# First expert's tokens gathered by TensorE with 0/1 matrices beside the sort through DRAM

## The chip, the core and the metric

The kernel runs on one core of a Trainium2 chip. A core has TensorE (PE, matrix products, with its weight loads shown apart as PEld), VectorE (DVE), ScalarE (ACT), GpSimd (POOL) and SyncE (SP, which here only issues transfers). The metric is the device time of one execution in microseconds, the median of several runs.

## What is computed

Causal attention with a decay (2 batches, 8 heads, 576 positions, 64 columns each), then a mixture of eight experts with one expert for each of the 1152 tokens, then a dense two-layer product. The part that matters here is the mixture:

```python
logits = x @ w_gate                                   # 1152 x 512 by 512 x 8
expert_idx = np.argmax(logits, axis=1)
gate_w = softmax(logits)[arange(N), expert_idx]
for i in range(N):                                    # at most 288 tokens an expert
    e = expert_idx[i]
    if counts[e] < capacity:
        disp[e, counts[e]] = x[i]; pos[i] = counts[e]; counts[e] += 1; keep[i] = True
y = np.einsum('ecf,efd->ecd', np.maximum(np.einsum('ecd,edf->ecf', disp, w1), 0.0), w2)
out[i] = gate_w[i] * y[expert_idx[i], pos[i]]         # 0 where not kept
```

Each expert has w1 of 512x1024 and w2 of 1024x512.

## The kernel before

Every engine has a program of its own, written out by hand, and runs it in order; semaphores join them. Each float32 product is made of three: operands are split into a high part in fp32r and the rest (`hi`, `lo`), and TensorE computes hi*hi, lo*hi and hi*lo (L704, L705 and L706, `expert_product`).

**Attention** leaves in `xl` (in SBUF) the rows of all heads and their share of the logits. The 1152 tokens lie in 10 tiles (`TILES`) of 128 or 64 tokens.

**Routing** (from L1081) is a chain of short VectorE instructions. `onehot` (L1091) marks each token's expert; TensorE counts with `tri_b` and `ones_b` how many tokens of each expert stand before each token (L678 to L683); from `bank(0)` and `bank(1)` VectorE works out `starts` (where each expert begins in the sorted order), `dest` (each token's sorted place) and `scale` (its gate, 0 if dropped). `r_dest` and `r_side` tell the others.

**Sorting through DRAM.** The 10 tiles of scaled rows `xr` are made by VectorE (even tiles, L1131) and ScalarE (odd, L862). GpSimd scatters each with an indirect DMA to its place in `x_scratch` (L438). When all ten have landed, SP reads them back as 9 tiles `x_sorted` (L371). TensorE transposes each with four matmuls (`sorted_t`, L693), and ScalarE or VectorE copies the result into `x_t`. Three tiles (`FIRST_T`) hold the first expert's 288 columns: they come first, are split into `xe` (hi by ScalarE at L888, lo by VectorE at L1157), and expert 0 starts. The other six are transposed one behind each output tile `m` of expert 0's first layer. While TensorE has nothing to do it runs `spin`, products of ones that nobody reads: 98 of them ahead of the first transposed tile (L494).

**Experts.** `expert(e)` runs 8 output tiles of the first layer with 12 matmuls each, then 96 matmuls of the second layer, in the order kk 0 to 3 over all four m, then m by m over kk 4 to 7. ScalarE and VectorE take each hidden tile out of PSUM (L905, L1149), split the next weights (`cut_hi`, L271; `cut_lo`, L278; chunk 3 is w2's second half of expert 0, 4 and 5 are w1 of expert 1), and make the next expert's `xe`. `cut_x_hi` and `cut_x_lo` read the expert's start from `starts` into a register first. After expert 0 GpSimd zeroes `y_t` (L444), for which the first `y_high` waits (`pads`).

## Time and profile before

| | us |
|---|---|
| median of 3 runs | 589.86 (588.75 to 591.75) |
| the profiled execution, device time | 588.54 |
| its span, first to last instruction | 586.7 |
| attention, and the routing's counts done | to 140.8 |
| expert 0's first matmul | at 169.96 |
| expert 1's first matmul | at 198.17 |

Times in the trace are counted from the span's start. "Idle before" of a group is the time its engine stood still just ahead of it, with the engine and instruction that ended the wait. Matmuls overlap, so that the time between two starts, and not the duration of one, is what a matmul costs.

### The profile page before, as it was taken

Reading aid. Unit: us, or ns where it says so; the run is one execution under the profiler, and the core shown is the slowest. Engines: PE = TensorE matmul, PEld = TensorE weight load, DVE = VectorE, ACT = ScalarE, POOL = GpSimd, SP = SyncE. Lnnn points to the kernel's source line nnn. Section 1 sums busy time; section 2 is a strip of 40 time slices with the busy share of each in tenths; the row PEclk is TensorE's granted clock in tenths of the full one; section 3 lists DMA queues with packets and bytes.
Section 4 is the critical chain, followed back from the end, with each engine's and each line's share of the span. In section 5 each row is a group of like instructions: output and inputs, shape, how many; then the busy total and the mean of one; then the engine's idle time right before and its main releaser. Section 6 shows DMA issues by size and latency. Waiting matters only on the chain.

```text
span 586.7 us, 9523 instructions
## 1 busy us (share of the span) xinstructions
PE 568.8 (97%) x3694; PEld 504.0 (86%) x3694; DVE 327.5 (56%) x648; ACT 286.3 (49%) x571; POOL 60.0 (10%) x65
## 2 busy tenths in 40 slices
PE   7999999999989999999999999989999999999993
PEld 3688888886469999999999999979999898999992
DVE  4777777876124584665747556776333534353432
ACT  4677777762125364463735446655232323333330
POOL 7311111100702400000000000000000200010001
PEclk8999999999999999999999999999999999999998
DMA  8996563120460444626355462642000100000001
GB/s 167 228 276 179 165 153 85 69 73 2 164 235 0 144 155 181 215 97 216 114 174 185 175 216 73 216 144 73 0 1 1 54 1 1 2 33 22 1 0 54
DMA packets 51212, 63.63 MB, mean 108 GB/s; under 512 B 30496, under 2 KB 30528, under 8 KB 51168
## 3 DMA queue, kind: packets, MB, share of 16 engines
q1 hardware_dynamic: 48272, 57.34, 31.8%
q0 software_dynamic: 1520, 4.77, 2.2%
q10 hardware_dynamic: 1376, 0.92, 0.6%
q8 instruction: 29, 0.48, 0.4%
q14 instruction: 15, 0.12, 0.1%
HBM read 58.25 MB, written 4.77 MB: 107 GB/s over the span
## 4 chain that ended last, share of the span: by engine, by line
PE 90%; DVE 3%; POOL 2%; DMA 2%; issue 1%; ACT 1%; SPq 0%; DVEq 0%; ACTq 0%
PE ps L704 12%; PE ps L705 12%; PE ps L706 11%; PE ps L778 6%; PE ps L779 6%; PE ps L780 5%; PE ps L761 5%; PE ps L763 5%; PE ps L762 5%; PE ps L533 4%; PE ps L515 4%; PE ps L558 3%; PE ps L552 3%; PE ps L502 2%; POOL x_scratch L438 2%
## 5 line engine op out<-in xcount | busy, mean ns | idle before, releaser
L278 DVE TENSOR_TENSOR slot<-stage,slot 128x1024 fp32r<-128x1024 f32 x80 | 95.4, 1221 | 21.1 <-ACT slot L271 20.9
L930 ACT ACTIVATE act_t<-ps,half 128x384 f32<-128x384 f32 x48 | 27.9, 582 | 115.1 <-PE ps L763 115.1
L271 ACT ACTIVATE slot<-stage 128x1024 fp32r<-128x1024 f32 x80 | 81.4, 1052 | 4.6 <-DMA stage<-in_moe_w_in_dram 2.6
L1205 DVE SCALAR_TENSOR_TENSOR act_t<-act_t 128x384 f32<-128x384 f32 x48 | 26.8, 559 | 98.6 <-ACT act_t L930 98.6
L704 PE MATMUL ps<-xe,slot 128*128 128x288 f32 x256 | 75.8, 296 | 0.3 <-DVE xe L1157 0.3
L705 PE MATMUL ps<-xe,slot 128*128 128x288 f32 x256 | 75.6, 295 | 0.0
L705 PE MATMUL ps<-hid,slot 128*128 128x288 f32 x256 | 75.6, 295 | 0.0
L706 PE MATMUL ps<-xe,slot 128*128 128x288 f32 x256 | 75.3, 294 | 0.0
L706 PE MATMUL ps<-hid,slot 128*128 128x288 f32 x256 | 75.3, 294 | 0.0
L704 PE MATMUL ps<-hid,slot 128*128 128x288 f32 x256 | 75.2, 294 | 0.0
L905 ACT ACTIVATE hid<-ps 128x288 fp32r<-128x288 f32 x64 | 26.4, 412 | 99.7 <-PE ps L706 98.8
L761 PE MATMUL ps<-y_t,slot 128*128 128x384 f32 x192 | 64.8, 338 | 0.0
L763 PE MATMUL ps<-y_t,slot 128*128 128x384 f32 x192 | 64.6, 336 | 0.0
L762 PE MATMUL ps<-y_t,slot 128*128 128x384 f32 x192 | 64.4, 335 | 0.0
L1149 DVE SCALAR_TENSOR_TENSOR hid<-ps,hid 128x288 fp32r<-128x288 f32 x64 | 29.1, 454 | 60.9 <-ACT hid L905 60.9
L778 PE MATMUL ps<-slot,g_t 128*128 128x512 f32 x144 | 56.7, 394 | 1.9 <-DVE g_t L1213 1.9
L779 PE MATMUL ps<-slot,g_t 128*128 128x512 f32 x144 | 56.6, 393 | 0.0
L780 PE MATMUL ps<-slot,g_t 128*128 128x512 f32 x144 | 56.0, 389 | 0.0
L704 PEld LDWEIGHTS ps<-xe,slot 128*128 128x128 f32 x256 | 48.3, 189 | 0.8 <-DVE xe L1157 0.8
L706 PEld LDWEIGHTS ps<-xe,slot 128*128 128x128 f32 x256 | 48.4, 189 | 0.0
L706 PEld LDWEIGHTS ps<-hid,slot 128*128 128x128 f32 x256 | 48.4, 189 | 0.0
L704 PEld LDWEIGHTS ps<-hid,slot 128*128 128x128 f32 x256 | 48.3, 189 | 0.0
(163 smaller groups left out, 1054.4 us busy)
## 6 DMA issues: line engine op xcount, KB each, us to landing
stage<-in_moe_w_dram SPq DMA_DIRECT2D x32, 1024.0 KB, 5.2
cb<-c_scratch SPq DMA_DIRECT2D x7, 576.0 KB, 4.0
x_sorted<-x_scratch SPq DMA_DIRECT2D x9, 258.0 KB, 5.0
q_nat<-in_q_dram SPq DMA_DIRECT2D x16, 128.0 KB, 3.6
v_nat<-in_v_dram SPq DMA_DIRECT2D x16, 128.0 KB, 4.0
stage<-in_moe_w_in_dram SPq DMA_DIRECT2D x2, 1024.0 KB, 5.3
stage<-in_moe_w_out_dram SPq DMA_DIRECT2D x2, 1024.0 KB, 5.9
stage<-in_moe_w_in_dram SPq DMA_DIRECT2D x4, 512.0 KB, 5.1
```

The source lines that it names most:

```text
L271: nc.scalar.activation(s[:, 0, at], stages[n_buf][:, at], ACT.Copy).then_inc(w_hi, 1)
L278: nc.vector.tensor_tensor(s[:, 1, at], stages[stage_of(g)[0]][:, at], s[:, 0, at].bitcast(F32), ALU.subtract).then_inc(w_lo, 1)
L704: mm(bank(b, CAP), hi, x[:, 0], start=first, stop=False)
L705: mm(bank(b, CAP), lo, x[:, 0], start=False, stop=False)
L706: return mm(bank(b, CAP), hi, x[:, 1], start=False, stop=last)
L761: mm(bank(j % 2, TC), hi, y_t[:, 0, kk, TC * c:TC * c + TC], start=(kk == 0), stop=False)
L762: mm(bank(j % 2, TC), hi, y_t[:, 1, kk, TC * c:TC * c + TC], start=False, stop=False)
L763: last = mm(bank(j % 2, TC), lo, y_t[:, 0, kk, TC * c:TC * c + TC], start=False, stop=(kk == KD - 1))
L778: mm(b, gh, hi, start=(j == 0), stop=False)
L779: mm(b, gh, lo, start=False, stop=False)
L780: last = mm(b, gl, hi, start=False, stop=(j == NJ - 1))
L1149: V.scalar_tensor_tensor(out=hid[:, m, 1], in0=bank(m % 4, CAP), scalar=0.0, in1=hid[:, m, 0].bitcast(F32), op0=ALU.max, op1=ALU.subtract) ...
```

## The change

Expert 0's tokens no longer come from DRAM. Four pieces replace that:

- `sel`: ten 128x288 matrices of 0 and 1, made by GpSimd with a comparison of `slot_f` (0 to 287 in a row) with `place0`, the token's place within expert 0 (`before` of expert 0, plus 4096 for tokens of other experts). `slot_f` is made by two GpSimd instructions at the program's start.
- `sx`: the rows of each tile times the gate, split into hi (ScalarE) and lo (VectorE), six buffers deep.
- TensorE multiplies them (`select`): 4 matmuls of 128x288 for each tile and part, 80 in all, into banks 4 to 7, which then hold expert 0's rows selected and transposed. The lo part of a tile is taken `SLAG` (4) tiles behind its hi part.
- ScalarE and VectorE split the four banks into `xe`.

The scaled rows `xr` are still made, between the pieces of `sx`; GpSimd's ten scatters stand behind its ten comparisons. All nine sorted tiles are now transposed within expert 0's second layer, at the places of `SORT_AT`, into banks 0 to 3. The cuts of chunk 3 stand behind hidden tiles 2 and 4, those of chunks 4 and 5 between the copies of sorted tiles, and expert 1's `xe` last. The zeroing of `y_t` is in two halves.

Core of the diff:

```diff
+SXR, SLAG = 6, 4
...
+        SORT_AT = {(1, 3): [0, 1], (2, 3): [2, 3], (3, 3): [4, 5], (7, 0): [6, 7], (7, 1): [8]}
...
             # GpSimd
+            step(g.iota(slot_i[:], pattern=[[1, CAP]], base=0, channel_multiplier=0))
+            step(g.tensor_copy(slot_f[:], slot_i[:]))
...
+            pool.wait_ge(places0, 2)
+            for i in range(TILES):
+                g.tensor_scalar(sel[:, i], slot_f[:], small[:, 10, i:i + 1], None, ALU.is_equal).then_inc(sel_sb, 1)
             pool.wait_ge(r_dest, 1)
...
+            pool.wait_ge(x0_ps, KD)
+            g.memset(y_t[:, 1].bitcast(F32), 0.0).then_inc(pads, 1)
             pool.wait_ge(xt_ps, ST)
             pool.wait_ge(idx_sb, 1)
-            g.memset(y_t[:].bitcast(F32), 0.0).then_inc(pads, 1)
+            g.memset(y_t[:, 0].bitcast(F32), 0.0).then_inc(pads, 1)
...
             # TensorE
+            spin(4, 3)
+            def select(i, part):
+                pe.wait_ge(sx_hi if part == 0 else sx_lo, i + 1)
+                if part == 0:
+                    pe.wait_ge(sel_sb, i + 1)
+                for kk in range(KD):
+                    last = mm(bank(4 + kk, CAP), sx[:, i % SXR, part, P * kk:P * kk + P], sel[:, i],
+                              start=(i == 0 and part == 0), stop=(i == TILES - 1 and part == 1))
...
+            for i in range(TILES + SLAG):
+                if i < TILES:
+                    select(i, 0)
+                if i >= SLAG:
+                    select(i - SLAG, 1)
...
-            spin(98, 3)
-            for t in range(FIRST_T):
-                sorted_t(t)
-                spin(4, 3)
-            spin(10, 3)
...
+                        if e == 0 and m == 0:
+                            pe.wait_ge(x0_lo, kk + 1)
...
-                    if e == 0 and FIRST_T + m < ST:
-                        sorted_t(FIRST_T + m)
...
+                    if e == 0:
+                        for t in SORT_AT.get((kk, m), []):
+                            sorted_t(t)
...
             # ScalarE
+            act.wait_ge(gates, 1)
+            for i in range(TILES):
+                select_hi(i)
+                if i in (4, 6, 7, 8, 9):
+                    scaled_rows({4: 1, 6: 3, 7: 5, 8: 7, 9: 9}[i])
...
+            for kk in range(KD):
+                act.wait_ge(x0_ps, kk + 1)
+                A.activation(xe[:, kk, 0], bank(4 + kk, CAP), ACT.Copy).then_inc(x0_hi, 1)
...
             # VectorE
+            V.tensor_scalar(off0, onehot[:, :, 0], -4096.0, 4096.0, ALU.mult, ALU.add).then_inc(places0, 1)
             then(V.reduce_sum(total, by_tile(expo), AX_X))
             then(V.tensor_scalar(total, total, 1.0e-9, None, ALU.add))
+            V.reciprocal(gate, total).then_inc(gates, 1)
...
+            V.tensor_tensor(place0, before.rearrange("p (t e) -> p t e", t=TILES)[:, :, 0], off0, ALU.add).then_inc(places0, 1)
...
-            V.reciprocal(gate, total).then_inc(r_side, 1)
...
+            for i in range(TILES):
+                select_lo(i)
+                if i % 2 == 0:
+                    scaled_rows(i)
+            for kk in range(KD):
+                dve.wait_ge(x0_hi, kk + 1)
+                V.tensor_tensor(xe[:, kk, 1], bank(4 + kk, CAP), xe[:, kk, 0].bitcast(F32), ALU.subtract).then_inc(x0_lo, 1)
...
                 if e == 0:      # ScalarE; VectorE has the like with tiles 1, 3, 5, 7
+                    cut_hi(4, 0)
+                    cut_hi(4, 1)
+                    sorted_copy(0)
+                    sorted_copy(2)
+                    cut_hi(5, 0)
+                    sorted_copy(4)
+                    cut_hi(5, 1)
+                    sorted_copy(6)
+                    sorted_copy(8)
+                    cut_x_hi(1)
+                    continue
```

TensorE, from the counts on, before (`xs_in0` is the landing of the first sorted tile):

```order
L683 MATMUL ps<-onehot,ones_b 128x8 x10
L494 MATMUL ps<-ones_b 128x512 x98
L693 MATMUL ps<-ident,x_sorted 128x128 [waits xl_sb,xs_in0]
L693 MATMUL ps<-ident,x_sorted 128x128 x3
L494 MATMUL ps<-ones_b 128x512 x4
```

and now:

```order
L699 MATMUL ps<-onehot,ones_b 128x8 x10
L510 MATMUL ps<-ones_b 128x512 x4
L709 MATMUL ps<-sel,sx 128x288 [waits sel_sb,sx_hi,xl_sb]
L709 MATMUL ps<-sel,sx 128x288 x3
L709 MATMUL ps<-sel,sx 128x288 [waits sel_sb,sx_hi]
```

In the place of 98 spins and the wait for DRAM stand four spins and the selecting matmuls, which wait for the comparisons and for `sx`.

VectorE behind the routing chain, before:

```order
L1127 CAST starts<-small 128x8
L1131 TENSOR_SCALAR xr<-xl,small 128x512 [waits r_side]
L1131 TENSOR_SCALAR xr<-xl,small 128x512 x4
L278 TENSOR_TENSOR slot<-stage,slot 128x1024 [waits w_hi,w_st0]
L278 TENSOR_TENSOR slot<-stage,slot 128x1024 [waits w_hi]
```

and now:

```order
L1190 CAST starts<-small 128x8
L1198 SCALAR_TENSOR_TENSOR sx<-xl,small,sx 128x512 [waits sx_hi]
L1206 TENSOR_SCALAR xr<-xl,small 128x512 [waits r_side]
L1198 SCALAR_TENSOR_TENSOR sx<-xl,small,sx 128x512 [waits sx_hi] x2
L1206 TENSOR_SCALAR xr<-xl,small 128x512
```

and so on to the tenth lo part. The five scaled rows now stand between ten lo parts, and the cuts of chunk 3 have moved into expert 0.

ScalarE after expert 0's last hidden tile, now (before, the cuts of chunks 4 and 5 stood behind `xe`, and the copies of sorted tiles in the first layer):

```order
L951 ACTIVATE hid<-ps 128x288 [waits h_ps] x3
L278 ACTIVATE slot<-stage 128x1024 [waits h_ps,w_st1]
L278 ACTIVATE slot<-stage 128x1024
L923 ACTIVATE x_t<-ps 128x4x128 [waits xt_ps] x2
L278 ACTIVATE slot<-stage 128x1024 [waits h_ps,w_st2]
L923 ACTIVATE x_t<-ps 128x4x128 [waits xt_ps]
```

against before:

```order
L905 ACTIVATE hid<-ps 128x288 [waits h_ps] x2
L887 TENSOR_LOAD starts [waits pads,xt_a,xt_v]
L887 ISA x2
L888 ISA
L888 ACTIVATE xe<-x_t 128x4x288
L271 ACTIVATE slot<-stage 128x1024 [waits h_ps,w_st1]
```

Expert 1's `xe` has moved behind the last sorted tile's copy.

## Rows read from the trace of the kernel before

**Rows 1.** The page: busy us, share of the span and instructions of each engine.

```profile
PE 568.8 (97%) x3694; PEld 504.0 (86%) x3694; DVE 327.5 (56%) x648; ACT 286.3 (49%) x571; POOL 60.0 (10%) x65
```

**Rows 2.** A stretch's busy us by engine, clock, DMA; then TensorE's waits (us, times, longest).

```profile
198.00:300.00 102.00, 102.00 (x774) 102.00 (x773) 61.84 (x72) 51.84 (x72) 0.00 (x0) 1.00 0.49 167
...
PE ps L778 <- DVE g_t L1213: 1.9, 2, 1.6
```

**Rows 3.** The chain that ended last, 140 to 170: start us, us, what.

```profile
140.81 0.18 DVE small L1105
...
145.32 1.25 POOL x_scratch L438
...
157.98 2.60 DMA x_scratch<-xr,dest
160.59 2.74 DMA x_sorted<-x_scratch
...
169.96 0.40 PE ps L704
```

**Rows 4.** TensorE in order of time: first matmuls of expert 1 and expert 2.

```profile
198.17 0.29 PE L704 MATMUL ps<-xe,slot 128*128 128x288 f32 x1
...
223.56 0.29 PE L704 MATMUL ps<-xe,slot 128*128 128x288 f32 x1
```

**Rows 5.** ScalarE and VectorE: two timeline rows, then groups (busy, mean ns | idle before).

```profile
143.85 3.18 ACT L862 ACTIVATE xr<-xl,small 128x512 f32<-128x512 f32 x5 [4.43 <-DVE starts L1127]
...
143.96 2.07 DVE L1131 TENSOR_SCALAR xr<-xl,small 128x512 f32<-128x512 f32 x5
...
L988 DVE TENSOR_TENSOR pt<-ps,pt 128x512 fp32r<-128x512 f32 x16 | 10.3, 684 | 0.0
...
L905 ACT ACTIVATE hid<-ps 128x288 fp32r<-128x288 f32 x64 | 26.4, 412 | 99.7 <-PE ps L706 98.8
...
L1149 DVE SCALAR_TENSOR_TENSOR hid<-ps,hid 128x288 fp32r<-128x288 f32 x64 | 29.1, 454 | 60.9 <-ACT hid L905 60.9
```

**Rows 6.** GpSimd's elementwise groups; the last with min/median/max ns.

```profile
L429 POOL CAST vs<-v_nat 128x640 fp32r<-128x640 f32 x8 | 5.7, 716 | 79.1 <-PE ps L552 58.2 <-DMA v_nat<-in_v_dram 20.8
...
L414 POOL CAST erank<-erank_i 128x80 f32<-128x80 int32 x1 | 1.3, 1325 | 0.1
...
L395 POOL CAST ident_b<-ident 128x128 bf16<-128x128 f32 x1 | 0.3, 289 | 0.1
...
L431 POOL TENSOR_TENSOR vs<-v_nat,vs x8: 1545/1549/2460, 14.6 to 110.9; 128x640 fp32r<-128x640 f32 x8
```

**Rows 7.** VectorE and GpSimd at work at once, two places in the timeline.

```profile
14.27 1.47 DVE L1017 TENSOR_TENSOR_SCAN xl<-sc,xl 16x576 f32<-16x576 f32 x1
...
14.62 2.46 POOL L431 TENSOR_TENSOR vs<-v_nat,vs 128x640 fp32r<-128x640 f32 x1
...
148.08 2.36 DVE L278 TENSOR_TENSOR slot<-stage,slot 128x1024 fp32r<-128x1024 f32 x2 [2.05 <-ACT slot L271]
...
148.17 1.96 POOL L438 DMA_INDIRECT x_scratch<-xr,dest  x1 [0.31 <-issue]
```

**Rows 8.** TensorE's first transposes and the wait ahead; that stretch as in rows 2.

```profile
8.71 1.30 PE L502 MATMUL ps<-ident,q_nat 128*128 128x128 f32 x5 [2.61 <-DMA q_nat<-in_q_dram]
...
8.00:12.00 4.00, 3.29 (x14) 2.60 (x15) 2.76 (x3) 2.28 (x4) 2.96 (x8) 0.57 1.19 160
```

**Rows 9.** Expert 1's `xe` in the timeline, and the copies of sorted tiles (min/median/max ns).

```profile
186.61 1.17 ACT L888 ACTIVATE xe<-x_t 128x1152 fp32r x1 [0.52 <-issue]
...
188.83 1.36 DVE L1157 TENSOR_TENSOR xe<-x_t,xe 128x1152 fp32r<-128x1152 f32 x1 [2.13 <-issue]
...
L869 ACT ACTIVATE x_t<-ps x5: 597/597/598, 164.1 to 182.5; 128x512 f32<-128x512 f32 x5
```

**Rows 10.** Reading back: SP's issues in the timeline, and from issue to landing.

```profile
160.59 4.48 SPq L371 DMA_DIRECT2D x_sorted<-x_scratch  x9
...
DMA to landing us min/median/max: 2.7/5.0/5.7
```

More of the change, by code:

```diff
@@ L692, in sorted_t @@
                 for kk in range(KD):
[L693 removed]
+                    last = nc.tensor.transpose(bank(t % 4, P, P * kk), x_sorted[:, t, P * kk:P * kk + P], ident[:])
                 last.then_inc(xt_ps, 1)
[L696 to L700 removed]
             def expert_product(b, hi, lo, x, first, last):
@@ L1075, in _ @@
             best, total, gate = row(3, TILES), row(4, TILES), row(5, TILES)
+            off0, place0 = row(9, TILES), row(10, TILES)
             pick9 = small[:, 6:8, :].rearrange("p a c -> p (a c)")[:, 0:TILES * (E + 1)].rearrange("p (t e) -> p t e", t=TILES)
```

124 lines of the change are left out of this document (76 added, 48 removed).

## The prediction

> **What bounds the kernel now.** The page first: TensorE is busy for 97% of the span, VectorE for 56% and ScalarE for 49% [rows 1]. That share has to be read by stage, since TensorE also spins there. From 198 us on it is really bound by its matmuls: it is busy for all of the 102 us after 198, and of all its waits behind that the view of waits lists 1.9 us [rows 2]. What brings expert 1 forward therefore brings the end forward by as much, as long as weights and splits keep up. The chain of waits then shows the one stage in which TensorE does nothing of use: the counts are out at 140.81, GpSimd scatters from 145.32 to about 158, the last scatter lands at 160.59, and expert 0 begins at 169.96 [rows 3]; between the first two the routing's chain ends at 143.96, where the scaled rows start [rows 5]. That is 29.15 us from the counts to expert 0, filled by spins.
>
> **Routing, now.** VectorE gets `off0` and `place0` ahead of its chain, some 0.15 us each, and loses the reciprocal from its middle. I count nothing: the chain still ends at about 143.96. The gate is ready by 140.9, so ScalarE starts `sx` hi at 141.0. GpSimd starts comparing at about 141.1.
>
> **Feeding the selection.** ScalarE: five scaled tiles took 3.18 us, and so (3.18 - 0.71) / 4 = 0.62 us each in a row [rows 5]. It has 10 hi parts and 5 scaled tiles; the tenth hi part is its 14th instruction, starts at 141.0 + 13 x 0.62 = 149.1 and ends at 149.8. VectorE: a scaled tile costs (2.07 - 0.48) / 4 = 0.40 us in a row. A 128x512 operation with two tensors takes 0.684 us [rows 5]; taking off the overlap of 0.08 that the scaled tiles show, 0.60 in a row. The tenth lo part starts at 143.96 + 9 x 0.60 + 5 x 0.40 = 151.4 and ends at 152.1. TensorE: 96 matmuls for a layer and 192 for an expert take 223.56 - 198.17 = 25.39 us [rows 4], 0.132 each, of the same 128x288 form. The 80 selecting ones are 10.6 us, 0.53 for a tile and part. With the interleaving, the last five groups follow the tenth hi part: 149.9 + 6 x 0.53 = 153.1. TensorE and VectorE end nearly together, at about 153.
>
> **GpSimd's comparison** is not in the trace: bounds. Below, its one-input rows: 0.289 us for 128 columns and 0.716 for 640 [rows 6], which is 0.83 ns a column and 0.42 us for 288. Above, by its two-input row, 1.549 for 640 [rows 6], 0.85 us with the same fixed part. The operation has one tensor, so I take 0.42: the tenth is done by 145.3. TensorE needs it at 149.9; it may take up to 0.88 us before it is late. The two new instructions at the start of the program lie ahead of work that has several microseconds of cover, and cost nothing.
>
> **GpSimd and VectorE in each other's way.** This is the term that I would have missed from durations alone. At 14.62 GpSimd's operation took 2.46 us for a usual 1.55, while VectorE was in a scan with two inputs from SBUF until 15.74; and the scatter at 148.17 took 1.96 us beside VectorE's subtraction at 148.08, which also reads two tensors from SBUF [rows 6, 7]. The lo parts of `sx` and some eight small steps of the routing chain read two tensors from SBUF, while GpSimd compares. Bounds: nothing, if only GpSimd gives way; and 2.6 us if each gives way to the other: eight steps wait for half a comparison (8 x 0.2 = 1.6) and the remaining two or three comparisons hold a lo part each (1.0). The first row is nearer to a full block of GpSimd (0.91 of the 1.12 us that the scan still ran); for VectorE it shows no clear loss. I take 1.5 us. The Trainium skill ("SBUF — State Buffer", section "SBUF: two separate sides") says that VectorE and GpSimd share a pair of ports under an exclusive lock, held for the whole instruction, and that the loser blocks fully. The trace agrees for GpSimd, with the 2.46 us; for VectorE no row decides. By the page the 2.6 us would hold, and the time would be 1.1 us above my forecast.
>
> **Into expert 0.** Behind the last selecting matmul of the first bank stand a ScalarE copy (0.41) and a VectorE subtraction (0.45) of 128x288 [rows 5], where there were copies of 1152 columns; the next three banks follow while TensorE computes. Without contention expert 0 runs as if begun at 153.1 + 0.9 = 154.0, against 169.96: 16.0 us. Contention takes it to 155.5.
>
> **Inside expert 0.** Before, expert 0 took 198.17 - 169.96 = 28.21 us, with six transposed tiles: (28.21 - 25.39) / 6 = 0.47 each. Now all nine are in it: 25.39 + 9 x 0.47 = 29.6. It costs 1.4 us, and matmuls end at 155.5 + 29.6 = 185.1.
>
> **The new wait.** Expert 1's `xe` now waits for the ninth sorted tile, which is transposed ahead of the last 24 matmuls. Behind it: the completion and ScalarE's copy, 0.15 + 0.60; the start's load, 0.52; hi, 1.17; from its end at 187.78 to VectorE's start at 188.83, with VectorE's own load, 1.05; lo, 1.36 [rows 9]. Together 4.9 us, against 24 x 0.132 = 3.2 of cover. TensorE stands still for 1.7 us (I hold 1.2 to 2.3 possible). Expert 1 begins at 186.8.
>
> **What stays hidden.** The scatters stand behind the comparisons and last 157.98 - 145.32 = 12.7 us to the last issue [rows 3]. With VectorE's lo parts in their way I let them begin at 147 and lose 2 more: the last lands at about 164.5, the first sorted tile at 167.2, the last at 164.5 + 4 + 5 = 173.5 [rows 10]. TensorE wants them at 155.5 + 12.7 + 3.2 = 171.4 and at about 181.5. 4 us of cover. Chunk 3's cuts are wanted at about 174; chunks 4 and 5 lie in the second layer, where ScalarE and VectorE have room.
>
> **The sum.** Selection instead of sorting -16.0; contention +1.5; three more transposed tiles +1.4; the wait before expert 1 +1.7: -11.4 us. From there on TensorE is the bound as before. Against the profiled execution, 588.54 (span 586.7), this gives 577.1; that execution lies 1.3 us under the median, and against the median of 589.86 it gives 578.5.
>
> **Rivals.**
> *The comparisons are slow.* If one takes 1.0 to 1.5 us (the two-input price of 0.85 plus blocks by VectorE), the tenth is done at 151 to 156.1, and TensorE still has 6 groups behind it: expert 0 is 0 to 5 us later, up to 583. For it: the bound is only twice what I take. Against: one tensor.
> *Sorted tiles late.* If the scatters are held up by over 4 us more than I count, the wait moves into the second layer: each us over it costs one; 580 to 584. For it: rows 7. Against: VectorE is through with lo parts at 153.
> *The clock falls.* The spins also kept TensorE at 2.4 GHz. Once it fell, to a mean of 0.57, after TensorE had stood still for 2.6 us at the start [rows 8]. If it ran at 1.2 GHz through the selection, 80 matmuls would take 21 us, and expert 0 would begin near 163.7: 586 to 587. Against: it gets 0.53 us of matmuls in each 0.62.
> *Slower than before.* One GpSimd row is out of line: a conversion of 80 columns took 1.325 us, 16.6 ns a column [rows 6]. A comparison at that price takes 4.8 us, the tenth ends at 189, and expert 0 begins at 193: 616. It decides from 2.2 us each, where the gain is gone. Against: that one broadcasts its input over ten short rows, and is the only one.
> *Nothing moves*, because something else holds expert 1 back to 198: no row speaks for it, as before its `xe` was ready 8 us ahead.
>
> **How the numbers follow.** Forecast 0.67, slow comparisons 0.13, late tiles 0.08, clock 0.04, slower 0.05, nothing 0.03. About 0.5% (3 us) is what a measurement can tell from no change here. The low end is no contention and a short new wait: 578.5 - 1.5 - 1.0 - 0.5 for the runs' spread, 575.5. The high end takes in slow comparisons and late tiles up to 583.5; what lies above holds less than 2 in 10. Faster 0.92, same 0.03, slower 0.05.
>
> **What would show it.** In the profile after: selecting matmuls from 141.7 to 153 or 155, at a clock of 1.0; the comparisons at 0.4 us each when alone, and VectorE's small steps stretched beside them; expert 0's first matmul at 154 to 156; a TensorE wait of 1 to 2 us for VectorE's `xe` before expert 1; none for `x_sorted`. A comparison of over 0.9 us, a wait at `x_sorted`, or a clock under 1 in the selection would make me wrong.

## The result and the profile after

| | before | after |
|---|---|---|
| median, us | 590.74 (588.75 to 593.09, 5 runs) | 584.35 (583.73 to 587.01, 5 runs) |
| the profiled execution, device time | 588.54 | 584.01 |
| its span | 586.7 | 581.9 |
| expert 0's first matmul | 169.96 | 157.64 |
| expert 0's second layer | 185.48 | 172.66 |
| expert 1's first matmul | 198.17 | 191.53 |
| expert 2's first matmul | 223.56 | 218.58 |

The ratio is 0.9915, 95% interval 0.9889 to 0.9941: about 0.9% faster. The time lies 5.9 us over the forecast of 578.5 and just above the range (575.5 to 583.5). A gain of 11.4 us was forecast, and 5.0 came through, read at expert 2. The difference to the prediction is therefore 6.4 us, and it has to be found ahead of 218.58. Behind it nothing is new: from expert 2's start to the end are 363.3 us, before 363.1.

The page of the kernel after, busy us by engine (to be held against [rows 1]):

```profile
PE 559.2 (96%) x3658; PEld 505.5 (87%) x3658; DVE 336.9 (58%) x663; ACT 292.6 (50%) x584; POOL 72.2 (12%) x78
```

GpSimd has 12.2 us more. The chain of waits of the kernel after, from the counts to expert 0 (start us, us, what; answers to [rows 3]):

```profile
140.73 0.16 DVE small L1168
...
140.98 4.78 POOL sel L445 x5
145.76 0.69 issue
146.45 5.60 POOL sel L445 x4
...
152.19 4.29 PE ps L709 x29
...
156.59 0.42 ACT xe L919
...
157.03 0.47 DVE xe L1215
...
157.64 0.37 PE ps L736
```

No transfer stands in this chain any more, and GpSimd's comparisons fill 10.4 us of its 16.9. The 0.69 us called "issue" is no pause: the fifth comparison is recorded from 144.93 to 146.47, and its increment of `sel_sb` at 146.48. The timeline of the same stretch (start us, busy us, instruction, idle time before and what ended it):

```profile
140.85 3.17 ACT L900 ACTIVATE sx<-xl,small 128x512 fp32r<-128x512 f32 x5 [1.44 <-DVE small L1159]
140.98 12.32 POOL L445 TENSOR_SCALAR sel<-slot_f,small 128x288 fp32r<-128x288 f32 x10 [28.54 <-DVE small L1168]
...
144.55 0.74 DVE L1198 SCALAR_TENSOR_TENSOR sx<-xl,small,sx 128x512 fp32r<-128x512 f32 x1
...
145.60 1.57 DVE L1198 SCALAR_TENSOR_TENSOR sx<-xl,small,sx 128x512 fp32r<-128x512 f32 x2
...
153.47 1.23 POOL L452 DMA_INDIRECT x_scratch<-xr,dest  x1 [0.17 <-issue]
```

The tenth comparison ends at 153.3 instead of the 145.3 that I had forecast, and behind it stand the six groups of matmuls of the interleaving and the two copies: expert 0 begins 4.34 us later. VectorE's first lo part starts at 144.55 instead of 143.96.

Then the stages of expert 0 and 1, of the kernel after (stretch, busy us by engine, clock, DMA share, GB/s; the rows are expert 0's first layer, its second layer with the wait, and expert 1):

```profile
157.64:172.66 15.02, 13.66 (x97) 13.02 (x98) 5.66 (x11) 4.60 (x10) 12.48 (x9) 1.00 0.62 206
172.66:191.53 18.87, 16.88 (x135) 16.64 (x133) 9.95 (x13) 8.37 (x11) 4.91 (x1) 1.00 0.67 230
191.53:218.58 27.05, 27.05 (x193) 27.05 (x193) 15.55 (x18) 12.95 (x18) 0.00 (x0) 0.94 0.41 133
```

An expert's layer is 96 matmuls, 12.7 us [rows 4]. The first layer took 15.02 and lost 2.3 (the same layer of expert 0 takes 12.76 in an execution shown below). The second layer's matmuls, with nine transposed tiles, end at 189.37, 16.71 us behind its start, of which 12.69 are its own and 4.02 the tiles': 0.45 each, as predicted. Expert 1 took 27.05 us where [rows 4] have 25.39; its clock shows why, 0.94 on average. Four places, then: the start of expert 0 (2.1 us late), its first layer (2.1 over the forecast, since its matmuls took 31.73 us in all instead of 29.6), the wait before expert 1 (0.5 over), and expert 1's own clock (1.7).

Expert 1's `xe` in the timeline of the kernel after:

```profile
186.36 0.60 ACT L923 ACTIVATE x_t<-ps 128x512 f32<-128x512 f32 x1 [1.86 <-PE ps L731]
...
187.89 1.18 ACT L935 ACTIVATE xe<-x_t 128x1152 fp32r x1 [0.93 <-ACT x_t L923]
...
190.12 1.36 DVE L1234 TENSOR_TENSOR xe<-x_t,xe 128x1152 fp32r<-128x1152 f32 x1 [5.00 <-issue]
...
191.53 0.40 PE L736 MATMUL ps<-xe,slot 128*128 128x288 f32 x1 [1.99 <-DVE xe L1234]
```

Between two matmuls' starts TensorE had a gap of 2.28 us here, and 1.1 us behind it the granted clock was 0.50 from 192.6 to 196.0.

### The profile page after: what moved, and what is told of

It is laid out like the page before. It is cut to its first block, busy times and chain, and to the rows that moved or that the text cites. A ratio compares the mean times of both kernels' runs of the same rounds, so it can differ in the third digit from the quotient of the medians.

```text
span 581.9 us, 9504 instructions
## 1 busy us (share of the span) xinstructions
PE 559.2 (96%) x3658; PEld 505.5 (87%) x3658; DVE 336.9 (58%) x663; ACT 292.6 (50%) x584; POOL 72.2 (12%) x78
## 4 chain that ended last, share of the span: by engine, by line
PE 89%; DVE 2%; POOL 2%; issue 2%; ACT 1%; DMA 1%; another core or an unknown queue 1%; SPq 0%; DVEq 0%; ACTq 0%
PE ps L736 11%; PE ps L737 11%; PE ps L738 11%; PE ps L813 6%; PE ps L814 6%; PE ps L815 6%; PE ps L796 5%; PE ps L798 5%; PE ps L797 5%; PE ps L549 4%; PE ps L531 4%; PE ps L574 3%; PE ps L568 3%; POOL sel L445 2%; PE ps L518 2%
## 5 line engine op out<-in xcount | busy, mean ns | idle before, releaser
L464 POOL DMA_INDIRECT out_dram<-o_sb,tok_sorted x9 | 9.0, 995 | 377.6 <-DVE o_sb L1283 376.7
L736 PEld LDWEIGHTS ps<-xe,slot 128*128 128x128 f32 x256 | 49.0, 191 | 4.4 <-DVE xe L1234 2.2
L737 PEld LDWEIGHTS ps<-xe,slot 128*128 128x128 f32 x256 | 48.6, 190 | 0.8 <-issue 0.8
L738 PEld LDWEIGHTS ps<-xe,slot 128*128 128x128 f32 x256 | 49.0, 192 | 0.0
## 6 DMA issues: line engine op xcount, KB each, us to landing
cb<-c_scratch SPq DMA_DIRECT2D x7, 576.0 KB, 3.7
```

Source lines behind the costliest of these rows:

```text
L736: mm(bank(b, CAP), hi, x[:, 0], start=first, stop=False)
L737: mm(bank(b, CAP), lo, x[:, 0], start=False, stop=False)
L738: return mm(bank(b, CAP), hi, x[:, 1], start=False, stop=last)
```

## The experiments

The result is the first of five series. Fifteen more runs make the other four, each on one chip beside the kernel before. Three of the runs are the kernel after again, since what a single execution shows turned out to matter. "First layer" below is always expert 0's.

### The half clock behind the wait

**Spins in the wait.** Nine products of ones, ahead of the wait for expert 1's `xe`:

```diff
             for e in range(E):
+                if e == 1:
+                    pe.wait_ge(xt_v, 3)
+                    spin(9, 1)
                 if e >= 1:
                     pe.wait_ge(xe_lo, e)
```

> Nine spins (about 1.9 us of products that nobody reads) stand ahead of TensorE's wait for expert 1's xe. In the changed kernel that wait lasted 2.2 us, behind it the granted clock was half for 3.4 us, and expert 1 took 27.05 us against 25.39 before. Theory clock: the standstill made the clock fall; with spins it stays at full, expert 1 takes 25.4, and the time is 1.7 us under the changed kernel's. Rival: the slow stretch belongs to expert 1's place in time or to its load, not to the standstill; the clock falls all the same and the time doesn't move (or rises by the spins that run over, at most 0.3).

Measured: 580.31 us (580.16 to 583.23, 4 runs), ratio 0.9842 (0.979 to 0.9894), span 578.1. The stretch behind the wait, in the kernel after (stretch, busy us by engine, clock, DMA share, GB/s):

```profile
192.60:196.00 3.40, 3.40 (x17) 3.40 (x16) 1.00 (x2) 1.35 (x2) 0.00 (x0) 0.50 0.00 0
```

and the same in the kernel with spins, where expert 1 is by then 2.2 us further:

```profile
192.60:196.00 3.40, 3.40 (x28) 3.40 (x27) 2.27 (x4) 1.79 (x4) 0.00 (x0) 1.00 0.00 0
```

17 matmuls at 1.2 GHz against 28 at 2.4. Expert 1 took 25.5 us (189.30 to 214.82). The spins shorten nothing, as expert 1 still waits for its `xe`; only the half clock is gone. The rest of the difference to 581.9 is the first layer, which took 12.80 here. By itself this execution does not show that the spins did it, since the kernel without them also runs without the half clock at times, as the next lines tell.

Whether the clock falls behind this wait differs between executions. Eleven of those profiled have a gap of 2.26 to 2.30 us there. In seven (the first of the kernel after, and `plain_pool`, `scatter_late`, `sel_split`, `price`, `plain_fourth`, `late_fourth` below) a half-clock stretch of 3.4 us begins within 1.1 us of the gap's end; in four (`sel_alone` and the three later ones of the kernel after) none does. In none of the six executions without the gap (`before`, `spin_wait`, `sort_early`, `best`, `slag2`, `best2`) is there one before expert 1. It is this count, seven of eleven against none of six, that ties the half clock to the gap. The length of the gap does not tell the seven from the four. So the wait costs some 2.2 us, and in more than half of the executions 1.7 on top.

### What sets expert 0's start

**Comparisons alone.** VectorE's first lo part waits for all ten comparisons:

```diff
             def select_lo(i):
+                if i == 0:
+                    dve.wait_ge(sel_sb, TILES)
                 dve.wait_ge(sx_hi, i + 1)
```

> VectorE's first lo part waits for all ten comparisons, so that no operation with two tensors from SBUF runs beside the last six. In the changed kernel the first four comparisons took 1.00 us each and the last six 1.42. Theory price plus contention: all ten take 1.0 us, the tenth ends at 151.0 instead of 153.3, and lo parts take 0.74 us each with none at 0.9 or 1.0. Rival price alone: the later ones still take 1.25 or more, from ScalarE or TensorE at work beside them. The time itself will be higher, as lo parts start at 151 and end at 159: expert 0 at about 160.5.

Measured: 588.45 us (one execution), expert 0 at 166.04 instead of the expected 160.5. Two half-clock stretches put it back: one from 135.7 to 142.5, ahead of the change, and one from 152.7 to 159.6, which began within TensorE's 5.11 us before the first lo part. GpSimd's prices are not touched by that. The comparisons of this kernel (count, ns least/median/most, first and last start):

```profile
L445 POOL TENSOR_SCALAR sel<-slot_f,small x10: 990/991/1015, 144.0 to 152.9; 128x288 fp32r<-128x288 f32 x10
```

and those of the kernel after:

```profile
L445 POOL TENSOR_SCALAR sel<-slot_f,small x10: 997/1262/1565, 141.0 to 152.0; 128x288 fp32r<-128x288 f32 x10
```

By itself a comparison takes 0.99 us, more than my upper bound of 0.85. In the kernel after the first four take 1.00 to 1.02 beside VectorE's short steps, and the six beside lo parts 1.24 to 1.56. The lo parts give way too: in `sel_alone` all ten took 0.74 to 0.75 us, in the kernel after up to 0.99:

```profile
L1198 DVE SCALAR_TENSOR_TENSOR sx<-xl,small,sx x10: 739/742/991, 144.5 to 153.7; 128x512 fp32r<-128x512 f32 x10
```

Together the ten take from 140.98 to 153.3, 12.3 us; in `sel_alone` they take 9.82, one behind the other. Contention costs some 2.4 us on the path. The rival is out: the fifth and sixth comparison of `sel_alone` ran beside TensorE's and ScalarE's work (up to 149.7 and 149.3), and took 0.99 too. The Trainium skill ("SBUF — State Buffer", section "SBUF: two separate sides") says that the loser of the shared ports waits for the whole instruction. The direction agrees, on both engines here; the losses are 0.25 to 0.57 us for a comparison and up to 0.25 for a lo part, and don't tell whether a block is ever a whole instruction long.

**What the price hangs on.** Twelve instructions on GpSimd where TensorE does not wait for it, twice six forms:

```diff
             pool.wait_ge(x0_ps, KD)
+            g.memset(y_t[:, 1].bitcast(F32), 0.0).then_inc(probe, 1)
...
+                        last = g.tensor_scalar(dst, src, one, None, ALU.is_equal)
...
+                        last = g.tensor_scalar(dst, src, 1.0, None, ALU.is_equal)
...
+                        last = g.tensor_scalar(dst[:, 0:144], src[:, 0:144], one, None, ALU.is_equal)
...
+                        last = g.tensor_scalar(dst[:, 0:72], src[:, 0:72], one, None, ALU.is_equal)
...
+                        last = g.tensor_copy(dst, src)
...
+                        last = g.tensor_scalar(dst, src, 1.0, None, ALU.mult)
```

> The changed kernel with twelve more GpSimd instructions, twice six forms one behind the other, at a place where TensorE does not wait for GpSimd (behind the zeroing of half of y_t, in expert 0's first layer): the comparison with its threshold from SBUF on 288, 144 and 72 columns, the comparison with a constant, a copy and a multiplication by a constant on 288 columns. Theory A, the price is per column: 0.99 us for 288, 0.50 for 144, 0.25 to 0.30 for 72, and the copy takes 0.42 as worked out from the conversion's rows. Theory B, a fixed price of the form with a threshold from SBUF: 144 and 72 columns take nearly as long as 288, and the comparison with a constant is shorter. Some of the twelve may be longer where VectorE works on two tensors beside them; the shorter of each pair counts.

Measured, in one execution, by line (L465 the form of `sel`, L467 with a constant, L469 and L471 with 144 and 72 columns, L473 the copy, L475 the multiplication):

```profile
L465 POOL TENSOR_SCALAR y_t<-y_t x2: 1013/1018/1022, 175.5 to 181.8; 128x288 fp32r<-128x288 f32 x2
...
L467 POOL TENSOR_SCALAR y_t<-y_t x2: 1914/1942/1969, 176.6 to 182.9; 128x288 fp32r<-128x288 f32 x2
...
L469 POOL TENSOR_SCALAR y_t<-y_t x2: 647/814/980, 178.6 to 184.9; 128x144 fp32r<-128x144 f32 x2
...
L471 POOL TENSOR_SCALAR y_t<-y_t x2: 463/782/1102, 179.7 to 185.6; 128x72 fp32r<-128x72 f32 x2
...
L473 POOL CAST y_t<-y_t x2: 425/426/428, 180.2 to 186.8; 128x288 fp32r<-128x288 f32 x2
...
L475 POOL TENSOR_SCALAR y_t<-y_t x2: 935/941/947, 180.7 to 187.3; 128x288 fp32r<-128x288 f32 x2
```

The copy of 288 columns takes 0.43 us, which is the 0.42 that I had worked out from conversions, to the hundredth. The interpolation was right, the kind of instruction was not: a multiplication by a constant on the same columns already takes 0.94, and the comparison 1.01. With 72, 144 and 288 columns it is 0.46, 0.65 and 1.01, about 0.28 us and 2.5 ns a column. Theory A holds in its main point (a price by the column) with a fixed part that it did not have. The Trainium skill ("GPSIMD Engine Reference", section "Engine selection") calls GpSimd's elementwise operations with one input roughly line-rate; the copy here is in keeping with it, the multiplication and the comparison on the same columns, at over twice the time, are not. The long ones of a pair, and both of L467, stand beside one of VectorE's subtractions of two tensors (1.22 us each) and are 0.3 to 0.95 longer; for the comparison with a constant this experiment therefore gives no price of its own.

**Split between two engines.** VectorE makes the five odd ones ahead of the rest of its chain:

```diff
-            for i in range(TILES):
+            for i in range(0, TILES, 2):
                 g.tensor_scalar(sel[:, i], ...)
...
             V.tensor_tensor(place0, ...)
+            dve.wait_ge(places0, 2)
+            for i in range(1, TILES, 2):
+                V.tensor_scalar(sel[:, i], slot_f[:], small[:, 10, i:i + 1], None, ALU.is_equal).then_inc(sel_v, 1)
```

> The five odd comparisons are made by VectorE, ahead of the rest of its routing chain, the five even ones by GpSimd. Theory (GpSimd's ten comparisons at 1.0 to 1.6 us set the start of expert 0): GpSimd is through at about 146.5, VectorE's five take 0.25 to 0.35 us each (1.2 to 1.8 us together) and put its chain back by that, and its lo parts become the bound: expert 0 begins at 155.0 to 156.0 instead of 157.6, and the time falls by 1.6 to 2.6. Rival (what VectorE gives away in its chain and its lo parts costs as much): expert 0 begins at 157 or later and nothing is gained. The wait before expert 1 stays at about 2.2 us.

Measured: 582.13 us (580.76 to 584.23, 4 runs), ratio 0.9881 (0.9848 to 0.9915); the kernel after beside it had 580.25. The rival was right. GpSimd was through at 146.4, but VectorE's five took 2.44 us, its first lo part started at 146.37, and TensorE stood still for 2.06 us until it was there. From 149.0 to 152.4 the clock was half, and expert 0 began at 158.18. The half clock explains a part of that: 13 matmuls of the selection went at 0.24 us each instead of 0.13, 1.4 us. Without it, by my estimate from these starts, expert 0 would begin near 156.8, still behind the 155.0 to 156.0 of the theory, as the last lo part ended only at 155.07. TensorE in the timeline of this kernel:

```profile
142.51 2.88 PE L710 MATMUL ps<-sel,sx 128*128 128x288 f32 x20 [0.76 <-ACT sx L901]
147.16 0.80 PE L710 MATMUL ps<-sel,sx 128*128 128x288 f32 x4 [1.78 <-DVE sx L1202]
```

and the stretch of the selection (columns as before; the clock is 0.90 on average):

```profile
141.00:158.00 17.00, 13.68 (x84) 12.40 (x82) 14.18 (x40) 10.64 (x18) 13.88 (x9) 0.90 0.10 39
```

So VectorE is the next bound close behind the comparisons; in the kernel after its last lo part ends at 154.4, 1.1 us behind the last comparison.

### The late hidden tiles of the first layer

**The kernel after once more:**

> The changed kernel as it is, profiled a second time. In its first profiled execution expert 0's first layer took 15.02 us and TensorE stood still for 2.3 us in it, because ScalarE was told of three finished hidden tiles some 5 us late; in four variants that layer took 12.8. Theory A, an event of that one execution: the first layer takes 12.7 to 12.8 us here, and the span is about 579.6 (581.9 - 2.3) with the half clock behind the wait for expert 1's xe, 577.9 without. Theory B, it belongs to this kernel: 15.0 again and a span near 582. In both, the ten comparisons take 1.0 us alone and 1.2 to 1.6 beside VectorE's lo parts, and expert 0 begins at 157.6.

Measured: 580.25 us (580.05 to 585.38, 4 runs), ratio 0.9873 (0.9828 to 0.9918), spans 578.1, 578.2, 578.2 and 583.3. ScalarE's second to fourth hidden tile in this execution:

```profile
161.11 0.41 ACT L951 ACTIVATE hid<-ps 128x288 fp32r<-128x288 f32 x1 [1.18 <-PE ps L738]
162.70 0.41 ACT L951 ACTIVATE hid<-ps 128x288 fp32r<-128x288 f32 x1 [1.18 <-PE ps L738]
...
164.28 0.41 ACT L951 ACTIVATE hid<-ps 128x288 fp32r<-128x288 f32 x1 [0.23 <-PE ps L738]
```

and the second to fifth in the first execution:

```profile
162.83 0.41 ACT L951 ACTIVATE hid<-ps 128x288 fp32r<-128x288 f32 x1 [2.92 <-issue]
167.85 0.41 ACT L951 ACTIVATE hid<-ps 128x288 fp32r<-128x288 f32 x1 [4.62 <-remote]
...
169.11 0.70 ACT L951 ACTIVATE hid<-ps 128x288 fp32r<-128x288 f32 x2
```

Here tiles come every 1.585 us and the first layer takes 12.76. In the first execution the third tile must have been finished near 162.7, too, since TensorE ran without a gap until 165.9; but its increment of `h_ps` is recorded at 167.83, with those of the next two behind it at 167.96 and 168.08. There is a second trace of it: ten scatters with sixteen increments each make 160 of `x_out`. This execution has all 160, the first one 48, and the last of the 48 is at 167.54, just ahead of the late increments (171.00 and 171.03 in `after_third`; but in `slag2` below the late ones come at 169.4 and the last of the scatters' at 170.3). The clock did not fall either, where I had expected it half behind the wait.

What TensorE itself lost in the first execution is mostly not a wait for a late hidden tile. Its longest gap there:

```profile
165.91 0.29 PE L738 MATMUL ps<-xe,slot 128*128 128x288 f32 x1
167.10 0.29 PE L736 MATMUL ps<-xe,slot 128*128 128x288 f32 x1 [0.90 <-issue]
```

and the one of `slag2`:

```profile
168.64 0.29 PE L738 MATMUL ps<-xe,slot 128*128 128x288 f32 x1 [0.80 <-issue]
```

The program waits for hidden tiles (`h_lo`) only ahead of a tile's twelve matmuls. These gaps lie between the third and fourth, and between the eleventh and twelfth, matmul of the sixth tile, where it waits for nothing. In the first execution two such gaps (1.19 and 0.46 between starts) cost 1.4 us; the gaps ahead of the seventh and eighth tile (0.33 and 0.56), where TensorE does wait for late hidden tiles, cost 0.6. In `price` and `slag2` one gap in the sixth tile (1.03 and 1.09) is nearly the whole loss. All five executions with a longer first layer have such gaps in that tile. So late increments and TensorE's standing still come together, but the one is not simply the cause of the other.

**And again, with two further series:**

> The changed kernel once more. So far its executions had spans of 581.8, 581.9, 582.3, 583.5 and 585.0 in one series, and of 578.1, 578.2, 578.2 and 583.3 in another. In the profiled 581.9 two things were found that the profiled 578.1 does not have: 2.3 us from hidden tiles that reached ScalarE late, and 1.7 us from a half-clock stretch behind the wait for expert 1's xe. Theory: these two come and go between executions, and a third series has spans near 578.1, 579.8, 580.4 or 582, each with its mean clock (0.994 without a half-clock stretch, 0.991 with one). Rival: two fixed levels that belong to a series, so that all of this one lie at 578 or all at 582.

Measured: 583.15 us (582.21 to 585.63, 4 runs), ratio 0.9877 (0.9846 to 0.9908), spans 583.6, 581.6, 580.6, 580.1. First layer 14.88 us, 60 increments. The profiled 583.6 also has a half-clock stretch from 136.3 to 143.1, ahead of anything changed, so that expert 0 began at 160.99.

> The changed kernel once more, as the one to which the next two are compared. In the executions whose first layer had late hidden tiles (15.0, 14.9, 13.8 and 13.9 us instead of 12.8) the trace holds 48 to 69 increments of the scatters' semaphore, in those without 160, sixteen for each scatter. Theory: the two go together, and this execution has either about 50 to 70 increments and a first layer of 13.8 to 15.0 us, or 160 and 12.8.

Measured: 582.0 and 584.89 us, ratio 0.9895 (0.9822 to 0.9968), profiled span 580.2. First layer 14.89 us, 59 increments. The two go together, as expected, and of the two theories on levels the rival comes nearer: the late tiles belong to a series. The second and third series had them in none of eight profiled executions, six of them with indirect scatters beside at least a part of the first layer; the first, fourth and fifth had them in all six with indirect scatters there, though one of the six (`best2`) lost no time by it. It isn't the chip: the third and the fifth series ran on the same one.

**Plain transfers in place of indirect ones:**

```diff
-                g.indirect_dma_start(out=x_dram[:, :], out_offset=bass.IndirectOffsetOnAxis(ap=dest[0:n, i:i + 1], axis=0),
-                                     in_=xr[0:n, i, :], in_offset=None).then_inc(x_out, 16)
+                row0 = P * i if i < NT else S + P * (i - NT)
+                pool.dma_start(x_dram[row0:row0 + n, :], xr[0:n, i, :]).then_inc(x_out, 16)
```

> The ten indirect scatters are replaced by ten plain transfers of the same rows on GpSimd's queue, in token order; all experts but the first then get other tokens' rows, and the amount of work is unchanged. In the changed kernel TensorE's increments for the second to fourth hidden tiles reached ScalarE only at 167.8, when the last scatter had landed, though its matmuls for the second ended near 162.7; expert 0's first layer took 15.0 us instead of 12.7. Theory scatter: the indirect transfers cause it; the first layer takes 12.7 and the time is 2.3 us lower. Rival any transfer: plain ones do the same, 15 us. Rival place: it is not the transfers but something at that place of TensorE's program, 15 us again, but not ending with the last landing.

Measured in the second series: 582.94 us (582.81 to 584.77, 4 runs), ratio 0.988 (0.9831 to 0.9928), expert 0 at 158.96 because a half-clock stretch from 136.4 to 139.9, ahead of anything changed here, moved all by 1.3 us. First layer 12.80, wait of 2.28 and half clock as in the first execution. At that time it told nothing about the late tiles, since that series had none. The same kernel in the fifth series:

> GpSimd's ten indirect scatters are plain transfers of the same rows, so that experts 1 to 7 get other tokens' rows. If the execution of the changed kernel beside it has the late hidden tiles: Theory A (the indirect transfers' increments hold back TensorE's) says that they are gone here, and expert 0's first layer takes 12.8 us; Theory B (any transfer issued by GpSimd does it) says 13.8 to 15.0 as there. If that execution does not have them, this one tells nothing.

Measured: 581.67 us (one execution), span 579.6. First layer 12.76 us, all 160 increments, in a series in which the kernel after had 14.89 and 59. ScalarE's second and third hidden tile:

```profile
161.04 0.41 ACT L951 ACTIVATE hid<-ps 128x288 fp32r<-128x288 f32 x1 [1.17 <-PE ps L738]
162.62 0.41 ACT L951 ACTIVATE hid<-ps 128x288 fp32r<-128x288 f32 x1 [1.17 <-PE ps L738]
```

**Scatters behind the first layer:**

```diff
             pool.wait_ge(r_side, 7)
+            pool.wait_ge(h_ps, KF)
             for i in range(TILES):
```

> GpSimd's ten scatters wait until expert 0's first layer is done, so that no scatter runs beside it. Theory scatter: the first layer takes 12.7 us with no late increments, and the lateness moves into the second layer or the wait for sorted tiles, of some 12 us or more. Rival place: the first layer takes 15 us though nothing is scattered, with increments late from the second tile on.

Measured in the second series: 598.46 us (one execution). First layer 12.76, the scatters from 171.42 to 183.14, and TensorE waited 15.1 us for the first sorted tile. Even then the half clock was back: 178.9 to 192.5.

> The scatters wait until expert 0's first layer is finished. If the execution of the changed kernel beside it has the late hidden tiles: by the theory that the scatters in flight hold back TensorE's increments the first layer takes 12.8 us here, while hidden tiles are taken late in no stage, since TensorE then waits for the sorted tiles anyway; by the rival (something else in expert 0's first layer, for instance the weights' transfers) it takes 13.8 to 15.0. If that execution does not have them, this one tells nothing.

Measured in the fifth: 598.73 us (one execution), first layer 12.77. Only 146 of the scatters' 160 increments are recorded, against all 160 in the second series, so that this series' loss of records is there while the first layer is not late. With the scatters out of it, TensorE's increments come in time; with plain transfers in it, too. That fits Theory A: indirect scatters in flight go with late increments, in some series. It is not proof. Each of the two deciding runs is a single execution, with one late one (`after_fourth`) beside it in its series. The plain transfers are also over sooner (last one issued at 158.19 instead of 165.03, last increment at 164.75), so that none of them was in flight from 165.7 on, where TensorE stood still in its sixth tile in `after_fourth`; the second and third hidden tile, though, were in time here while plain transfers were in flight. Why only some series have it, by which way it comes about, why TensorE stands still in the middle of a tile, and whether the recording of the profile has a part in it, are open. The kernel before scattered in every series while TensorE only spun, and nobody waited for an increment of TensorE: its profile has 98 of the 160 increments, and yet the span of 586.7 is the least, or within 0.3 us of it, in every series.

### Versions made of the findings

**Sorted tiles earlier:**

```diff
-        SORT_AT = {(1, 3): [0, 1], (2, 3): [2, 3], (3, 3): [4, 5], (7, 0): [6, 7], (7, 1): [8]}
+        SORT_AT = {(1, 3): [0, 1], (2, 3): [2, 3, 4], (3, 3): [5, 6, 7, 8]}
```

> Sorted tiles 6 to 8 are transposed some 5 us earlier, in the part of expert 0's second layer with kk 0 to 3, so that the copies and expert 1's xe come earlier by as much. Theory (the wait for xe costs its 2.2 us and, behind it, 1.7 us of half clock): no wait before expert 1 and no half clock; expert 1 begins at about 187.1 if expert 0 begins at 157.6 and its first layer takes 12.8; span about 575.8, 3.9 us less than the kernel after without the late hidden tiles. Rival 1 (the sorted tiles are not there yet): the last x_sorted lands near 177, and TensorE waits for it in the second layer, up to 2 us. Rival 2 (the copies' banks are the bound): TensorE waits for a bank that ScalarE or VectorE has not emptied, and the gain is under 2 us.

Measured: 578.15 us (577.78 to 579.46, 4 runs), ratio 0.9815 (0.9787 to 0.9843), span 576.0; expert 1 at 187.34, its `xe` ready at 186.73 and no wait. In the timeline of this kernel:

```profile
183.16 1.17 ACT L935 ACTIVATE xe<-x_t 128x1152 fp32r x1 [1.40 <-DVE x_t L1219]
...
185.37 1.36 DVE L1234 TENSOR_TENSOR xe<-x_t,xe 128x1152 fp32r<-128x1152 f32 x1 [3.01 <-issue]
```

Neither rival came: no wait for `x_sorted` and none for a bank. Against the kernel after beside it (span 578.1, without half clock) it is 2.1 us, nearly the whole wait of 2.26 between starts.

**Both edits:**

> Both edits together: sorted tiles earlier, and the comparisons split between GpSimd and VectorE. If each gain stands by itself the span is near 573.8 and the time 5.5 to 6.5 us under that of the kernel after without late hidden tiles, about 575; ratio to the kernel before 0.973. Rival: expert 0 begins 2 us earlier but the sorted tiles do not, so that TensorE waits for x_sorted in the second layer and the sum is less than the two parts, near 577.

Measured: 578.36 us (577.86 to 579.68, 5 runs), ratio 0.9816 (0.9792 to 0.984): nothing over the earlier sorted tiles alone. The 2.07 us of standing still and the half clock behind it (150.0 to 153.4) are here as in the split alone.

**Lo parts two tiles behind instead of four** (`SXR, SLAG = 6, 2`, with the earlier sorted tiles):

> On top of the earlier sorted tiles: the lo part of a tile is multiplied two tiles behind its hi part instead of four, so that behind the last comparison (153.3) stand four groups of 0.53 us instead of six. Theory (expert 0 starts at the last comparison plus what stands behind it): expert 0 begins at 156.6 instead of 157.7, span 574.9. Rival (VectorE's last lo part, which ends at 154.4, is the bound): the last group can start at 154.5 at the earliest, which is the same 155.0 and leaves the gain at 1.1; if TensorE's longer wait for the first lo part cannot be made up, the gain is under 0.5.

Measured: 579.5 us (578.11 to 579.56, 4 runs), ratio 0.9813 (0.9782 to 0.9843). The selection did as expected: TensorE began it 1.4 us later than in `sort_early` (half clock from 136.8 to 140.2, ahead of the change), expert 0 only 0.4 later, at 158.22, so 1.0 us was won. The first layer took 13.89 us, in a series with late tiles (69 increments), and took it back. By the rival the gain was to be 1.1 or under, by the theory 1.1: the two are not told apart.

**Three comparisons on VectorE, seven on GpSimd**, with the earlier sorted tiles, the lo parts three tiles behind, and each scaled row of VectorE behind the next lo part:

```diff
-            for i in range(TILES):
+            for i in (0, 1, 3, 4, 6, 7, 9):
                 g.tensor_scalar(sel[:, i], ...)
...
+            for i in (2, 5, 8):
+                V.tensor_scalar(sel[:, i], slot_f[:], small[:, 10, i:i + 1], None, ALU.is_equal).then_inc(sel_v, 1)
...
                 select_lo(i)
-                if i % 2 == 0:
-                    scaled_rows(i)
+                if i % 2 == 1:
+                    scaled_rows(i - 1)
```

> On top of the earlier sorted tiles: VectorE makes three comparisons (tiles 2, 5, 8) ahead of its chain, GpSimd seven, the lo parts run three tiles behind, and each of VectorE's scaled rows stands one lo part later. At the measured 0.49 us each VectorE gives away 1.5 us; GpSimd is through at 149.4. Theory (with the comparisons out of the way VectorE is the bound): its last lo part ends at 154.2 to 154.5, expert 0 begins at 155.8 to 156.2, span 574.2 to 574.5. Rival (TensorE's wait for the first lo part is followed by half clock, as it was when VectorE made five): expert 0 begins at 157 or later and nothing is gained over the earlier sorted tiles alone (span 576.0).

Measured: 576.32 us (575.92 to 579.79, 6 runs), ratio 0.9788 (0.9757 to 0.982), span 574.0; the best of all, while the kernel after beside it had 583.15 (with late tiles, and a half-clock stretch in its profiled execution). In its own six, two have spans of 577.7 and 577.8. From its chain of waits (start us, us, what):

```profile
140.82 1.41 DVE sel L1175 x3
...
145.55 0.66 DVE sx L1205
...
146.26 8.39 PE ps L713 x61
...
154.76 0.42 ACT xe L923
```

From 146.26 on TensorE itself is the bound, with no gap until its last selecting matmul. Its wait for the first lo part was 1.49 us, and the clock did not fall. The first layer took 12.77 although the series has late tiles: only 80 increments are recorded, and those of the fourth to sixth hidden tile stand close together (165.56 to 165.81; the fourth was finished near 162.4). TensorE has no gap in its sixth tile here. Its last scatter was issued at 163.25 instead of 165.11; whether that is the reason is not shown.

## Why the prediction was wrong, point by point

Four steps failed. The comparison and its contention were priced too low (0.42 and 1.5 us; 0.99 and 2.4 measured), which makes 2.1 us of the 6.4. "Inside expert 0" has only transposed tiles, and nothing for the scatters that now run beside the first layer: 2.1, cause in part open. "The new wait" was put at 1.7 (2.16 measured): 0.5. Nothing was put for the clock behind that wait: 1.7. A comparison of over 0.9 us was one of my own signs of being wrong, and it came.

**The bound and the mechanism** were read rightly. Expert 0 was waiting for the sort, experts are bound by TensorE, and what brings expert 2 forward brings the end forward by as much: 4.98 us there, 4.8 in the span.

**The comparison was mis-sized** ("The operation has one tensor, so I take 0.42"). It takes 0.99. I had interpolated conversions of one tensor, and the copy of 288 columns measures 0.43, as worked out; but a multiplication or comparison with a scalar costs over twice as much a column. With 0.99 the tenth is done at 150.9, and with 4.34 us behind it expert 0 would begin at 155.2 instead of 154.0: 1.2 us, since it is over my threshold of 0.88. I had this case as the rival "slow comparisons", at 0.13. The 0.85 of the nearest row with two tensors was no upper bound, since it was another operation as well. It was also worked out wrongly: with the fixed part that [rows 6] give, 0.18 us, it is 0.80.

**Contention was mis-sized**, 1.5 taken and 2.4 measured. The mechanism was right, in both directions. It is larger because six of the slow comparisons run beside lo parts, where I had counted two or three. 154.0 + 1.2 + 2.4 = 157.6.

**The new wait** was 2.16 us behind the last matmul (2.28 between starts) instead of 1.7: between the copy of the ninth tile and ScalarE's hi part stand 0.93 us, where [rows 9] had 0.52. That was within my 1.2 to 2.3.

**The clock behind the wait** was missing. I had looked for a fall in the selection, where TensorE has short gaps, and not behind the one gap of about 2 us that I had forecast myself, though [rows 8] show half clock behind 2.61 us. It cost 1.7 us in the profiled execution, and came in six of the ten others with that wait. For that gap, the cost is read from the rows (27.05 against 25.39 us for expert 1); why it comes in some and not in others is open.

**The first layer** has no term in the sum at all for what it lost, 2.1 us. Moving the scatters beside it was priced by duration and landing only. What the runs show in its place is 1.4 us of TensorE standing still in the sixth tile, where the program has no wait, and 0.6 of waits for hidden tiles that ScalarE took late; both come only with indirect scatters in flight, and not in every series. No row of before could show it, as TensorE only spun there.

**Right** were: the routing chain's end but for 0.6 us of contention, the transposed tiles at 0.45 us, the sorted tiles in time (they landed at 170.4 to 177.5, 3 to 4 us behind the forecast 167.2 and 173.5, but TensorE wanted the first at 175.8 and the last at 185.7), chunk 3's cuts, and the clock in the selection, 1.0.

The sum: 2.1 + 2.1 + 0.5 + 1.7 = 6.4 us of the 11.4. The last and the second come and go, and so do half-clock stretches near 136 us; the same kernel has spans from 578.1 to 585.0. Without all three it is at 580.05 to 580.31 us, inside the range, and still about 2 over the forecast, since the slow comparisons and the longer wait are in every execution. The range had been widened upward for slow comparisons.

## What to carry to other kernels

Price an instruction by a row of the same operation on the same engine; a row with the same shape and fewer operands is another instruction, and the "upper bound" from a dearer-looking one may lie below it. When a sum forecasts that TensorE will stand still for 2 us, count the clock behind it too, or move the producer earlier rather than filling the wait: here it was worth 2.1 us, and no half clock was seen with it. And when transfers move beside a new stage, read every gap of that stage against the waits in the program: one where the program waits for nothing has another cause. Profile more than one execution, in more than one series, before a loss in one of them is given a cause.

## What the runs showed of the hardware

- GpSimd: a copy of 128x288 takes 0.43 us, a multiplication by a constant 0.94, a comparison with a column of SBUF 1.01 (0.65 for 144 columns, 0.46 for 72). VectorE makes the same comparison in 0.37 to 0.61, five in 2.44.
- With indirect scatters of GpSimd in flight, TensorE's increments for finished tiles reached ScalarE up to 5 us late (recorded at 167.83 for a tile finished near 162.7), in three series of five; not with plain transfers, and not with the scatters later (one execution each in such a series). In five of the six executions that have it TensorE also stood still for 1.0 to 1.4 us within its sixth tile, where the program has no wait.
- Behind gaps of 2.06 to 2.30 us TensorE's granted clock was half (1.2 GHz) for 3.4 us in nine of thirteen cases. Behind 1.49 and 1.88 us (once each, the latter in the kernel before at 161.49) and behind the 1.94 to 2.05 us at 369 to 392 us, which every execution has, it never was. In waits of 5.1 and twice 15.1 us it fell within the wait, all three times.
- A half-clock stretch came without a gap, too: in six executions for 3.4 or 6.8 us from about 136 us on, where TensorE has no gap over 0.6 us between starts from 100 to 140, is busy for all of 120 to 136, and nothing was changed. It moves all that follows by 1.3 or 3.3 us.
